# Key sums moved beside state products, scores in quarters, and a reordered start of a linear-attention and two-MoE kernel

## What is computed

```python
for t in range(S):                      # _attn_ref: 8 heads of 48
    cur = np.einsum('bhd,bhe->bhde', u[None] * kt, vt)
    y[:, :, t] = np.einsum('bhd,bhde->bhe', rt, state + cur)
    state = w[None, :, :, None] * state + np.einsum('bhd,bhe->bhde', kt, vt)
...
return (silu * val @ w_out)             # _moe_ref: gate, value, out; 1536 hidden
...
out[mask] = gate_w[mask, None] * eom[mask, e, None] * ye   # _moe2_ref: one of 8 experts each, 1024 hidden
```

## Time and profile before

| | |
|---|---|
| runs shown | 875.5 us median of 3 (875.4 to 878.33) |
| the profiled execution, its own time | 873.72 us |
| its span, first to last instruction | 871.9 us |
| mean granted TensorE clock | 0.992 |
| TensorE busy | 845.8 us, 97% |
| VectorE / ScalarE / GpSimd busy | 64% / 37% / 20% |

### The profile page before, as it was taken

One profiled execution on the slowest core, in us unless ns is written; L12 is line 12 of the kernel. 1 busy time (PEld: TensorE's weight loads), 2 busy tenths in 40 slices (PEclk: granted clock), 3 DMA queues, 4 the chain that ended last, 5 costly groups with the idle time before them and its releaser, 6 DMA issues. The chain is left out here.

```text
span 871.9 us, 19225 instructions
## 1 busy us (share of the span) xinstructions
PE 845.8 (97%) x7523; PEld 736.5 (84%) x7523; DVE 559.2 (64%) x1131; ACT 319.4 (37%) x522; POOL 172.9 (20%) x139
## 2 busy tenths in 40 slices
PE   7799999999999999999999999999899999999995
PEld 5578887788878888788777878899899999999995
DVE  7667746673666456744564446459969777887770
ACT  3422331112211131113111221347458666677651
POOL 2223203250233213230322001003111101111010
PEclk9899999999999999999999999999999999999999
DMA  9235301131122102220101002537986679666700
GB/s 351 103 112 200 132 1 57 58 116 35 37 78 94 57 1 78 92 94 1 58 23 38 1 1 65 227 136 244 381 304 258 233 251 327 254 250 248 275 17 19
DMA packets 23711, 115.66 MB, mean 133 GB/s; under 512 B 3324, under 2 KB 9392, under 8 KB 18016
## 3 DMA queue, kind: packets, MB, share of 16 engines
q1 hardware_dynamic: 19408, 98.96, 31.4%
q0 software_dynamic: 3520, 9.87, 3.0%
q10 hardware_dynamic: 720, 5.90, 2.0%
HBM read 101.63 MB, written 14.16 MB: 133 GB/s over the span
## 5 line engine op out<-in xcount | busy, mean ns | idle before, releaser
L1594 PE MATMUL bank<-X1H,WH 128*128 128x512 f32 x432 | 169.8, 394 | 1.1 <-DVE X L978 0.8
L1594 PE MATMUL bank<-X1L,WH 128*128 128x512 f32 x432 | 169.0, 392 | 0.1
L1594 PE MATMUL bank<-X1H,WL 128*128 128x512 f32 x432 | 168.8, 392 | 0.0
L771 ACT ACTIVATE SG<-bank 128x512 f32<-128x512 f32 x72 | 43.1, 599 | 250.2 <-PE bank L1594 250.2
L1207 DVE TENSOR_TENSOR TT<-bank,SG 128x512 f32<-128x512 f32 x72 | 49.8, 691 | 125.1 <-ACT SG L771 124.5
L683 ACT ACTIVATE AH<-PP 128x512 fp32r<-128x512 f32 (+1 forms) x78 | 46.1, 598 | 159.7 <-DVE PP L1212 159.7
L1594 PEld LDWEIGHTS bank<-X1H,WH 128*128 128x128 f32 x432 | 81.7, 189 | 19.3 <-issue 2.1
L1594 PEld LDWEIGHTS bank<-X1H,WL 128*128 128x128 f32 x432 | 81.6, 189 | 17.6 <-DVE WL L1031 0.3
L1594 PEld LDWEIGHTS bank<-X1L,WH 128*128 128x128 f32 x432 | 81.6, 189 | 17.1 <-DVE X1L L1037 0.5
L1640 PE MATMUL bank<-AH,WH 128*128 128x512 f32 (+1 forms) x234 | 91.7, 392 | 0.0
L1215 DVE TENSOR_TENSOR AL<-PP,AH 128x512 fp32r<-128x512 f32 (+1 forms) x78 | 57.5, 743 | 50.9 <-ACT AH L683 50.9
(11 more groups left out here) (220 smaller groups left out, 1814.2 us busy)
## 6 DMA issues: line engine op xcount, KB each, us to landing
W_EVEN<-w SPq DMA_DIRECT2D x20, 1536.0 KB, 8.2
W_ODD<-w SPq DMA_DIRECT2D x18, 1536.0 KB, 8.3
RK_IN<-unit_rk SPq DMA_DIRECT2D x20, 736.0 KB, 4.5
V_IN<-unit_v SPq DMA_DIRECT2D x20, 448.0 KB, 3.3
STG<-w_dense ACTq DMA_DIRECT2D x5, 1152.0 KB, 5.5
XG_ODD<-store SPq DMA_DIRECT2D x9, 394.0 KB, 8.5
store<-PAD SPq DMA_DIRECT2D x8, 394.0 KB, 4.5
RK_START<-unit_rk SPq DMA_DIRECT2D x4, 512.0 KB, 6.2
```

Source lines behind the costliest of these rows:

```text
L771: nc.scalar.activation(SG[:, :], GATE_PS[:, :], ACT.Sigmoid).then_inc(sig_ready, 1)
L1594: last = mm(bank_[:, :], lhs[:, f, m, k * P:k * P + P], rhs[:, k, :], start=(x == 0), stop=(x == len(terms) - 1))
```

## The change

TensorE does the key sums inside outputs, right behind the state products, in the odd slices; the wait for gate_free moves with them, and gate_sums_used is awaited one slice later. The state terms get columns of bank 5 in place of bank 7, so scores wait for the state of the unit before. Scores are split: 64 keys by all 128 queries, and the other 64 keys by the later 64 queries; the mask is applied in the same two parts. decay_state and the sum become four scalar_tensor_tensor instructions. The routing steps of blocks 1 to 4 go from f = 1, 3, 5 to f = 2, 4, 6. In block 0 the sigmoid of f = 0 comes first on ScalarE, then load_dense(1), and the states of sequences 2 and 3 come after AH. At the start the constants are loaded behind the first r and k; VectorE makes POWR alone and ScalarE copies it reversed into POWK; the 22 transposes become 7 products of 384 columns; both receptances are scaled ahead of both keys. GpSimd's order becomes k, r, rk, kt. The diff, cut to what matters (indentation cut by eight; left out are two semaphore declarations and two waits that change their name):

```diff
@@ -277,7 +277,7 @@
         self.scores = self.y = bank[5], bank[6]
-        self.c_banks, self.u = (bank[7], bank[0]), bank[7]
+        self.c_banks, self.u = (bank[7], bank[0]), bank[5][:, PAIRS * VW:2 * PAIRS * VW]
         self.rk, self.v = RK_IN[self.odd], V_IN[self.odd]
@@ -435,7 +435,6 @@
     sp.dma_start(CST[:, C_W:C_ID], consts[:, C_W:C_ID]).then_inc(decays_loaded, 16)
-    sp.dma_start(CST[:, C_ID:C_ALL], consts[:, C_ID:C_ALL]).then_inc(consts_loaded, 16)
 
@@ -446,7 +445,7 @@
         if u.last:
-            sp.wait_ge(r_scaled, u.i + 1)
+            sp.wait_ge(rxk_scaled, u.i + 1)
         else:
@@ -466,6 +465,8 @@
             sp.dma_start(u.rk[:, :], unit_rk[u.i, :, 0:I_KT]).then_inc(u.rk_sem, 16)
+            if u is u0:
+                sp.dma_start(CST[:, C_ID:C_ALL], consts[:, C_ID:C_ALL]).then_inc(consts_loaded, 16)
         for u in some:
@@ -607,9 +608,10 @@
     def scale_unit(u):
-        scale_rk(u)
+        u.wait_rk(pool)
         scale_k(u)
         scale_r(u)
+        scale_rk(u)
         if not u.last:
@@ -618,17 +620,18 @@
     u0, u1, u2, u3 = [Unit(0, b) for b in range(BATCH)]
-    pool.wait_ge(r_start_scaled, 3)
+    pool.wait_ge(k_start_scaled, 3)
...
-    scale_rk(u4)
+    u4.wait_rk(pool)
+    scale_r(u4)
     pool.wait_ge(keys_turned, BATCH - 1)
     scale_k(u4)
-    scale_r(u4)
+    scale_rk(u4)
     pool.wait_ge(dense_low, 3)
@@ -719,6 +722,8 @@
     act.wait_ge(decay_ready, 1)
+    copy(POWK[:, :, :], POWR[:, :, ::-1]).then_inc(decay_turned, 1)
+    act.wait_ge(decay_turned, 1)
     for j in range(PAIRS):
@@ -733,8 +738,8 @@
     turned_keys(3)
-    for b in range(BATCH):
-        first_state(b)
+    first_state(0)
+    first_state(1)
 
@@ -758,10 +763,7 @@
             act.wait_ge(value_ready, FT * n)
-        if first:
-            act.wait_ge(dense_low, 3)
-            load_dense(1)
-        else:
+        if not first:
             x1_highs(n)
@@ -769,6 +771,9 @@
             nc.scalar.activation(SG[:, :], GATE_PS[:, :], ACT.Sigmoid).then_inc(sig_ready, 1)
+            if first and f == 0:
+                act.wait_ge(dense_low, 3)
+                load_dense(1)
             if f >= 2:
@@ -794,6 +799,8 @@
                 if f == 0:
+                    first_state(2)
+                    first_state(3)
                     act.wait_ge(y_ready, BATCH)
@@ -944,27 +951,28 @@
         c.step(tt(WPOW[:, :, x + 1:x + 2], WPOW[:, :, x:x + 1], WPOW[:, :, x:x + 1], ALU.mult))
-    nc.vector.reciprocal(POWR[:, :, 0:1], WPOW[:, :, 6:7])
-    c.step(nc.vector.reciprocal(POWK[:, :, P - 1:P], WPOW[:, :, 6:7]))
+    c.step(nc.vector.reciprocal(POWR[:, :, 0:1], WPOW[:, :, 6:7]))
     for x in range(7):
         m = 2 ** x
         power = WPOW[:, :, x:x + 1].broadcast_to([PR, PAIRS, m])
-        if x == 4:
+        if x == 5:
             key_products(u0)
-        tt(POWR[:, :, m:2 * m], POWR[:, :, 0:m], power, ALU.mult)
-        c.step(tt(POWK[:, :, P - 2 * m:P - m], POWK[:, :, P - m:P], power, ALU.mult))
+        c.step(tt(POWR[:, :, m:2 * m], POWR[:, :, 0:m], power, ALU.mult))
...
-    def first_scales(u):
+    def scale_first_r(u):
         u.wait_rk(dve)
         need(dve, scores_ready, 2 * u.i - 2 if u.i >= 2 else 0)
+        tt(u.rw[:, :], u.rk[0:PR, I_R:I_R + PAIRS * P], POWR[:, :, :].rearrange("p j t -> p (j t)"),
+           ALU.mult).then_inc(r_start_scaled, 1)
+
+    def scale_first_k(u):
+        dve.wait_ge(decay_turned, 1)
         need(dve, keys_turned, u.i - 1 if u.i >= 2 else 0)
         tt(u.kw[:, :], u.rk[0:PR, I_K:I_K + PAIRS * P], POWK[:, :, :].rearrange("p j t -> p (j t)"),
            ALU.mult).then_inc(k_start_scaled, 1)
-        tt(u.rw[:, :], u.rk[0:PR, I_R:I_R + PAIRS * P], POWR[:, :, :].rearrange("p j t -> p (j t)"),
-           ALU.mult).then_inc(r_start_scaled, 1)
 
@@ -987,18 +995,21 @@
             dve.wait_ge(scores_ready, 2 * u.i + half + 1)
-            tt(u.am[:, half, :, :], u.scores[half][:, :].rearrange("p (j t) -> p j t", j=PAIRS),
-               mask.unsqueeze(1).broadcast_to([P, PAIRS, P]), ALU.mult).then_inc(masked, 1)
-
-    def decay_state(u):
-        dve.wait_ge(y_ready, u.i + 1)
-        dve.wait_ge(state_ready, u.i - 3)
-        tt(ST[:, u.b, :, :], ST[:, u.b, :, :], WPOW[:, :, 7:8].broadcast_to([PR, PAIRS, VW]), ALU.mult)\
-            .then_inc(decayed, 1)
+            made = u.scores[half][:, :].rearrange("p (j t) -> p j t", j=PAIRS)
+            strict = mask.unsqueeze(1).broadcast_to([P, PAIRS, P])
+            if u.first:
+                last = tt(u.am[:, half, :, :], made, strict, ALU.mult)
+            else:
+                tt(u.am[EARLIER, half, :, :], made[EARLIER, :, :], strict[EARLIER, :, :], ALU.mult)
+                last = tt(u.am[LATER, half, :, LATER], made[LATER, :, LATER], strict[LATER, :, LATER], ALU.mult)
+            last.then_inc(masked, 1)
 
     def add_output(u):
-        dve.wait_ge(y_ready, u.i + 1)
         dve.wait_ge(c_used, u.i + 1)
+        if u.first or u.last:
+            dve.wait_ge(y_ready, u.i + 1)
+        else:
+            dve.wait_ge(u_ready, u.i + 1)
         if u.first:
@@ -1011,13 +1022,13 @@
         dve.wait_ge(u_ready, u.i + 1)
-        dve.wait_ge(decayed, u.i - BATCH + 1)
-        tt(ST[:, u.b, :, :], u.u[0:PR, 0:PAIRS * VW].rearrange("p (j e) -> p j e", j=PAIRS), ST[:, u.b, :, :],
-           ALU.add).then_inc(state_ready, 1)
+        dve.wait_ge(state_ready, u.i - BATCH + 1)
+        for s in range(PAIRS):
+            last = stt(out=ST[:, u.b, s, :], in0=ST[:, u.b, s, :], scalar=WPOW[:, s, 7:8], in1=u.u[0:PR, s * VW:s * VW + VW],
+                       op0=ALU.mult, op1=ALU.add)
+        last.then_inc(state_ready, 1)
 
     def finish_unit(u):
-        if not u.last:
-            decay_state(u)
         add_output(u)
@@ -1037,10 +1048,13 @@
 
-    first_scales(u0)
-    first_scales(u1)
+    scale_first_r(u0)
+    scale_first_r(u1)
+    scale_first_k(u0)
+    scale_first_k(u1)
     key_products(u1)
-    first_scales(u2)
+    scale_first_r(u2)
+    scale_first_k(u2)
     mask_scores(u0)
@@ -1228,20 +1242,20 @@
             if not first:
-                if f == 1:
+                if f == (1 if last else 2):
                     copy_logits(n)
-                if f == (2 if last else 3):
+                if f == (2 if last else 4):
                     copy_turned_logits(n)
-                if f == (3 if last else 5):
+                if f == (3 if last else 6):
...
-                    own_key(u)
                     mask_scores(u)
                 else:
+                    own_key(u)
                     finish_unit(u)
@@ -1454,10 +1468,6 @@
         pe.wait_ge(c_used, u.i)
-        if not isinstance(u.i, int):
-            pe.wait_ge(state_ready, u.i)
-        elif u.i > BATCH:
-            pe.wait_ge(state_ready, min(u.i, UNITS - BATCH))
         pe.nop(nofuse=True)
@@ -1494,10 +1504,18 @@
                 pe.wait_ge(kh_copied, BATCH)
+            else:
+                pe.wait_ge(state_ready, min(u.i, UNITS - BATCH) if isinstance(u.i, int) else u.i)
+            pe.nop(nofuse=True)
         for s in range(PAIRS):
             for x in range(2):
                 a = Head(PAIRS * x + s)
-                last = mm(u.scores[x][:, a.keys], u.kw[a.rows, a.keys], u.rw[a.rows, a.keys], start=True, stop=True)
+                to, w, r = u.scores[x][:, a.keys], u.kw[a.rows, a.keys], u.rw[a.rows, a.keys]
+                if u.first:
+                    last = mm(to, w, r, start=True, stop=True)
+                else:
+                    mm(to[EARLIER, :], w[:, EARLIER], r, start=True, stop=True)
+                    last = mm(to[LATER, LATER], w[:, LATER], r[:, LATER], start=True, stop=True)
                 if s == PAIRS - 1:
@@ -1525,6 +1543,7 @@
                 opened.add(at)
+            key_sums(u)
         u.wait_v(pe)
@@ -1537,10 +1556,9 @@
             pe.wait_ge(masked, 2 * BATCH - 2)
-            need(pe, c_used, BATCH if u.b >= 2 else 0)
+            pe.wait_ge(c_used, BATCH if u.b >= 2 else 2)
         else:
             pe.wait_ge(kt_scaled, u.i + 1)
-        pe.wait_ge(c_used, u.i + 1)
         for s in range(PAIRS):
@@ -1550,8 +1568,8 @@
     pe.wait_ge(consts_loaded, 16)
-    for x in range(22):
-        nc.tensor.transpose(bank[2][:, 0:P], ident, ident)
+    for x in range(7):
+        mm(bank[2][:, 0:3 * P], ident, CST[:, C_ID:C_ID + 3 * P], start=True, stop=True)
     u0, u1, u2, u3 = [Unit(0, b) for b in range(BATCH)]
@@ -1703,28 +1721,28 @@
             need(pe, gate_free, q)
-            if f == 2 and not first:
+            if f == (2 if last else 3) and not first:
                 pe.wait_ge(logits_copied, n)
-            if f == (3 if last else 4) and not first:
+            if f == (3 if last else 5) and not first:
                 pe.wait_ge(logits_read, n)
-            if f == (4 if last else 6) and not first:
+            if f == (4 if last else 7) and not first:
                 pe.wait_ge(ranks_copied, n)
-            if f % 2 == 1 and f // 2 < len(units):
```

(14 more changed lines are left out.)

6 lines of the change are left out of this document (3 added, 3 removed).

## The result

The changed kernel takes 903.17 us, median of 4 runs (902.71 to 910.58), beside 875.45 us (874.95 to 878.33): ratio 1.0329, 95% interval 1.0272 to 1.0387. 866.0 was forecast, with 872.5 as the high end. The profiled execution has a time of 902.71 and a span of 900.5, against 873.72 and 871.9: 29 us more.

The account below looks back on a forecast made before the run. TensorE, busy 97% of the span, was taken as the bound. From 873.72 us the terms -3.0 - 1.0 + 1.5 - 1.6 - 5.8 + 2.0 = -7.9 gave 865.8, said as 866; range about 861.5 to 872.5.

Parts of the forecast that it names:

- the move of the routing: Blocks 1 to 3: routing in even slices and no decay put VectorE 0.2 us ahead of TensorE at f = 5.
- merged groups: Key sums joined to state products in one group of 8 rounds, 1.04 us in place of 0.60 + 0.60.
- The rival with 0.06: TensorE starves for instructions between state products and values in 20 units; at 0.75 us each +15, 881; chance 0.06.
- The quarters: Scores of 20 units on four tiles: shorter first weight load, 0.05 us each, -1.0; bounds -4.4 and +8.8.
- the rounds: Small matmuls of different array tiles start together, every 0.11 us at 128 columns; taken as evidence against quarters in series.
- VectorE's mask: Mask of a unit on VectorE goes from 1.20 us to 1.86, with two more instructions of some 0.33 each.
- The stop at f = 4: TensorE's stop at f = 4 of blocks 1 to 3 goes, some 0.53 us each: -1.6 (-2.2 to 0).
- Key sums beside state products: One group of 1.04 us saves 0.16 for each unit; 19 x 0.16 = -3.0.
- start +2.0: Kernel's start: later warm-up puts outputs at 17.5 for 14.28, +3.2, with 1.2 given back: net +2.0 (0 to +4).
- sigmoid -5.8: Block 0, sigmoid first on ScalarE: outputs of f = 1 start at 40.6 and not 46.81, counted as -5.8.
- stops +1.5: Block 0, f = 3, 5, 7: TensorE waits for TT, a new stop of 0.5 us each: +1.5 (0 to 2.4).
- rival 1: Block 0: clock falls anyway around the 2.3 us stop, price 3.6 us, about 869.5; chance 0.25 together with another rival.

Follow-up runs that it names:

- late sends: Changed kernel with GpSimd's record sends of blocks 1 to 4 held back until the last unit's outputs are done: 880.0 us, 1.0044.
- whole scores: Scores and mask made whole again, quarters undone: in the changed kernel 893.11 us, 1.0191; in the kernel with late sends 873.29 us, 0.9969.
- the kernel with the lowest time: Kernel with late sends and whole scores, with the start undone and 128 empty instructions ahead of everything on TensorE: 868.12 us, 0.9909.

## Why the prediction was wrong

**The step that failed.** Part by part, the move of the routing was costed for VectorE only: "With the decay gone and routing moved to even slices, I count VectorE as 0.2 us ahead of TensorE at f = 5". Behind positions hang four indirect DMAs of GpSimd, and they moved with it, from a short burst of f = 6 and the dense products behind it into the long burst of f = 7. "Reordering GpSimd (k, r, rk, kt) and SyncE's waits costs nothing" weighed the multiplications, and no sentence the sends. Their price there is 23 us (late sends), and 22 the other way round in the kernel before. For blocks 1 to 4 the sum had 5.0 us less (sixteen merged groups and sixteen scores, and the stop at f = 4); measured are 26.4 more. Late sends take 23.8 off these blocks, and whole scores another 5.9.

**The rival with 0.06 was the right one, at the wrong place.** It had TensorE starve in its odd bursts, "in each of 20 units", at 0.75 us each: 15 us in all. It happened in one slice of four blocks, 5.1 us in block 1 (7.6 for 2.5), 5.5, 5.3 and 4.5 in the others, and the fallen clock behind it. "Against: no such stop stands behind steady bursts" was true, but the one burst of the kernel before with sends beside it was the short one of f = 6; what stands beside a burst, and how long the burst is, were the things to compare. In a smaller form the rival also held at f = 5 of blocks 1 to 3: these bursts last 1.3 to 1.7 us longer, by a stop in the state terms. The Trainium skill, Runtime: NRT & Kernel Launch, Instruction fetch mechanics, says that an engine's sequencer fetches its program in blocks of 256 instructions while it runs, and that the crossing is mostly hidden. In that stop, from 176 to 178.7, the only transfer of the core is one packet of instructions:

```profile
q8 instruction: 1, 0.02, 2.2%
```

That the packet causes the stop isn't shown. Most bursts have such a packet in them and don't stop, as with late sends the one of f = 7 in block 2 (286.70 to 289.24, packet at 287.26), which agrees with "mostly hidden". In that kernel block 1 has no stop at f = 5, and its packet comes at 177.75, behind the burst; blocks 2 and 3 have both. The cause of this stop stays open. Nor do such packets explain the slowing beside the sends: one lies in it in the kernel after, at 193.9, and none in the kernel before with its sends in the burst, where the first comes at 197.8.

**The quarters** did what their sum said on TensorE (1.03 measured, 1.04 forecast, -1.2 for -1.0), and did not run in series, so the rounds were right, and the rule on row groups of the Trainium skill (TensorE: Matmul & The Clock Gate, The mechanism) did not hold for these tiles. The term that was mis-sized is VectorE's mask: 56.43 to 58.73, 2.3 us, where 1.86 stood, since the two instructions of half the rows last 0.67 and 0.43, one after the other, 1.15 for each half of the heads where the whole was 0.60. AL ahead of it took 1.53 (54.90 to 56.43) for 1.19 in the kernel before; GpSimd multiplies beside it in both, so why it is longer stays open. Together they gave stops of 1.5 us, not of 0.5: +4.4 for the forecast +1.5. Costed at nothing was that the quarters double the matmuls and weight loads of scores. In the kernel before, the quarters alone cost 8.6 us, through the sends beside the longer burst of f = 6.

**The stop at f = 4** did go, but -1.6 didn't come: with the quarters' mask and route() ahead of TT, TensorE waits 0.78 at f = 5. Without quarters blocks 1 to 3 are 0.9 to 1.2 us shorter. The sum had 0.64 of that from four merged groups; the rest, 0.3 to 0.5, is what came of the 0.53 for this stop.

**Key sums beside state products** were nearly right: 0.44 + 0.64 = 1.08 at f = 3 of block 0, forecast 1.04, as one group for two of 0.60. That saves 0.12 for each unit, where 0.16 stood.

**Block 0** was forecast to begin block 1 some 2.8 us earlier (start +2.0, sigmoid -5.8, stops +1.5, three merged groups -0.5); it began 2.2 later. The start was right in size: the state terms of f = 0 begin at 34.08 for 31.80, +2.3, though by another way. The warm-up ended at 12.0, forecast 13.0, but the first dense products met X1L beside GpSimd, 2.52 us for two where 1.1 is usual, and a wait of 1.7. The sigmoid was right: the outputs of f = 1 start 42.86 - 34.08 = 8.8 us later, and the stop is 2.35, forecast 2.3. In the kernel before alone it gave 5.6 for 5.8. What is off are the stops for TT, 2.9 of the 5.0, and the clock: rival 1 came true too, it was granted at 1.2 GHz for 3.4 us from 43.3, and key sums, values and state terms took 3.7 us where they take 2.1. Its price in the prediction was a little low for the kernel before: by the earlier trace rows the fall there cost 2.7 us in f = 1 and 1.4 in key sums and scores, not 1.0.

## What to carry to other kernels

When a step is moved, follow it to the last instruction that hangs on it, on every engine, and ask what each of those will lie beside: here a routing step on VectorE carried four DMAs of GpSimd into TensorE's longest run of short instructions. Count the instructions of such a run: with the sends beside it, 48 pairs of load and matmul got through and 64 did not, and splitting products to save columns makes more of them. A wait that lets only two indirect sends be under way bought back 22 us here, without knowing where the burst is; and of a change with seven parts, one alone (the sigmoid first) gave 5.6 us, where the kernel with the lowest time gains 7.6.

## What the hardware showed that was not expected

- Three or four indirect sends of GpSimd, queued from a block's first on, cut TensorE to ten instructions in 0.73 us, where 256 take 2.5 us undisturbed. Two, or the last three, or 0.81 MB by a plain DMA, do nothing.
- It shows once 44 to 52 pairs of load and matmul of the burst are through, and lasts in the kernel after until 0.7 to 0.8 us after the end of the fourth send (1.2 to 1.5 with whole scores); what decides is whether a third is free to follow, though it hasn't started.
- In each slowed burst of the kernel after the granted clock fell to 1.2 GHz, in block 1 for 3.4 us from 196.9, in block 2 for 6.8 us from 295.9.
- A stop that makes the burst of f = 5 longer by 1.3 to 1.7 us falls in the same place of three blocks (state terms). It is gone with whole scores, 16 matmuls and 16 loads fewer per unit, or when the burst is cut; with late sends it is in two of the three blocks.
- Quarters of 64 rows of output share rounds with those on the same input rows: 32 matmuls in 1.03 us.
